# Own terms and keys computed a tile ahead, powers of 1/w beside the squares, another home for half of the rows, smaller gate groups

## The reference

```python
# attention: B=2, H=8 heads, S=768, D=48
for t in range(S):
    cur = np.einsum('bhd,bhe->bhde', u[None] * kt, vt)
    y[:, :, t] = np.einsum('bhd,bhde->bhe', rt, state + cur)
    state = w[None, :, :, None] * state + np.einsum('bhd,bhe->bhde', kt, vt)
# experts: N=1536 tokens of 384, E=8, F=1024
expert_idx = np.argmax(x @ w_gate, axis=1)      # slot = number of earlier tokens of the same expert
h = np.maximum(np.einsum('ecd,edf->ecf', disp, w1), 0.0)
y = np.einsum('ecf,efd->ecd', h, w2)            # out[i] = gate * y[expert, slot]
# last: h = x @ w_in; solu = h * softmax(h); layer norm; @ w_out
```

## Time and profile before

| | us |
|---|---|
| median of 3 runs (lowest, highest) | 366.83 (365.44, 366.9) |
| profiled execution, whole | 366.17 |
| its span (first to last instruction) | 364.4 |
| busy: PE, DVE, ACT, POOL | 330.9, 200.9, 194.0, 189.9 |
| first product of expert 0 | 115.14 |

### The profile page before, as it was taken

The page is one execution under the profiler, slowest core; times in us unless marked ns, Lnnn a source line. Parts: engine busy times, 40 slices in busy tenths (PEclk is TensorE's granted clock), DMA queues, the critical chain, the costliest instruction groups (busy, mean ns, idle before and its releaser), DMA issues.

```text
span 364.4 us, 6469 instructions
## 1 busy us (share of the span) xinstructions
PE 330.9 (91%) x2390; PEld 290.8 (80%) x2390; DVE 200.9 (55%) x444; ACT 194.0 (53%) x372; POOL 189.9 (52%) x170
## 2 busy tenths in 40 slices
PE   5599997886758999999999999999899999999992
PEld 2388886775415999999999999977799999999992
DVE  4346644643362455564546556479966666665640
ACT  2365744756302768666676866645644444444430
POOL 6674757762176758869797885960111111111131
PEclk9879998998858999999999999999999999999998
DMA  8968879991029619485674949400000000000001
GB/s 147 270 191 216 249 178 274 285 345 44 20 82 233 192 27 322 155 289 178 207 247 148 338 142 318 188 4 0 3 22 23 22 22 23 22 23 22 23 25 40
DMA packets 62833, 50.64 MB, mean 139 GB/s; under 512 B 42448, under 2 KB 58192, under 8 KB 62800
## 3 DMA queue, kind: packets, MB, share of 16 engines
q1 hardware_dynamic: 58864, 45.25, 41.1%
q0 software_dynamic: 1920, 4.73, 3.5%
q10 hardware_dynamic: 2016, 0.21, 0.5%
HBM read 38.37 MB, written 11.82 MB: 138 GB/s over the span
## 4 chain that ended last, share of the span: by engine, by line
PE 72%; DVE 7%; issue 6%; POOL 5%; DMA 4%; ACT 4%; SPq 0%; POOLq 0%; DVEq 0%; ACTq 0%
PE ps L1143 23%; PE ps L1393 14%; PE ps L1379 11%; PE ps L1144 11%; PE ps L1402 3%; ACT scores L648 2%; PE ps L1270 2%; PE ps L1285 2%; DMA v_in<-in_v_dram 2%; DMA x_slots<-place,slot 2%; PE ps L1242 1%; PE ps L1265 1%; DMA rows_in<-x_slots 1%; PE ps L1137 1%; POOL place L507 1%
## 5 line engine op out<-in xcount | busy, mean ns | idle before, releaser
L438 POOL TENSOR_TENSOR w_lo<-w_raw,w_hi 128x768 fp32r<-128x768 f32 x32 | 58.6, 1858 | 23.0 <-DVE w_lo L444 22.9
L1143 PE MATMUL ps<-xe,w_hi 128*128 128x448 f32 x192 | 61.7, 377 | 0.3
L1143 PE MATMUL ps<-h,w_hi 128*128 128x448 f32 x192 | 61.6, 377 | 0.0
L1393 PE MATMUL ps<-w_hi,h 128*128 128x384 f32 x192 | 51.8, 340 | 0.3 <-issue 0.3
L1144 PE MATMUL ps<-h,w_lo 128*128 128x224 f32 x192 | 50.8, 264 | 0.0
L1144 PE MATMUL ps<-xe,w_lo 128*128 128x224 f32 x192 | 50.8, 264 | 0.0
L1379 PE MATMUL ps<-w_hi,xe 128*128 128x512 f32 x144 | 46.5, 392 | 0.5 <-DVE xe L1046 0.5
L816 DVE TENSOR_TENSOR ps<-ps,rk_in 128x448 f32<-128x448 f32 x32 | 20.2, 632 | 37.8 <-ACT rk_in L606 37.8
L1143 PEld LDWEIGHTS ps<-xe,w_hi 128*128 128x128 f32 x192 | 36.0, 187 | 5.3 <-issue 2.6
L444 POOL TENSOR_TENSOR w_lo<-w_raw,w_hi 128x1024 fp32r<-128x1024 f32 x16 | 38.2, 2406 | 1.9 <-DVE w_lo L444 1.9
L1143 PEld LDWEIGHTS ps<-h,w_hi 128*128 128x128 f32 x192 | 36.0, 188 | 2.6
(11 more groups left out here) (143 smaller groups left out, 661.0 us busy)
## 6 DMA issues: line engine op xcount, KB each, us to landing
w_raw<-in_moe_w_dram SPq DMA_DIRECT2D x16, 1536.0 KB, 7.6
x_slots<-zeros SPq DMA_DIRECT2D x6, 768.0 KB, 5.0
rk_in<-in_r_dram SPq DMA_DIRECT2D x12, 192.0 KB, 3.0
rk_in<-in_k_dram SPq DMA_DIRECT2D x12, 192.0 KB, 3.6
v_in<-in_v_dram SPq DMA_DIRECT2D x12, 192.0 KB, 4.2
out_dram<-zeros SPq DMA_DIRECT2D x1, 2304.0 KB, 13.5
rows_in<-x_slots SPq DMA_DIRECT2D x8, 192.0 KB, 7.6
w_raw<-in_moe_w_in_dram SPq DMA_DIRECT2D x1, 1536.0 KB, 6.1
```

The costliest lines, as they stand in the source:

```text
L438: eng.tensor_tensor(w1_lo[:, :, cols], w1_raw[:, i, :, cols], w1_hi[:, :, cols].bitcast(F32), ALU.subtract).then_inc(g.w1_lo, 1)
L1143: pe.matmul(ps[:, bank, 0:2 * n], w_hi, x[:, c, 0:2 * n], start=first, stop=False, skip_group_check=True)
L1393: last = pe.matmul(ps[:, OB + i, 0:DM], ht[:, f, i * P:(i + 1) * P], wt[:, f, :], start=(f == 0 and z == 0), stop=(f == KF - 1 and z == 2))
```

## The change

1. r and k of a tile have a semaphore without v; v has its own.
2. POOL does keys (`last_keys`) and own terms (`own_parts`) of tile t+1 in step t, with the state's decay between them, and the scatters behind them. DVE sums the own terms of tile t+2 at the end of step t. ACT writes the diagonal of t+1 before it copies the keys of t+1, and takes x last. The diagonal has a count for each half of the heads.
3. `wsq` also holds powers of 1/w, each the reciprocal of a square; `wpow` starts at 1/w and doubles downwards, in one loop with the squares.
4. Rows of x of batch 1 lie in the second w2 buffer, so taking x waits for no scatter. That buffer's first load moves behind the rows of experts 0 and 1.
5. Groups are tiles 0-2, 3-5, 6-8, 9, 10, 11; two scatters at most per step, from four steps after a group's last tile. Group 4 is counted before the last split of x. One part of w1 is rounded in each of the last four steps instead of two in two.
6. DVE does the routing sums before its remainders of w1, and these wait until all scatters are issued (`scatters_issued`).

```diff
+        def x_rows(t):
+            return x_first[:, t, :] if t < NC else w2_raw[:, 1, t - NC, :]
...
-        GROUPS = [range(0, 4), range(4, 8), range(8, 11), range(11, 12)]
+        GROUPS = [range(0, 3), range(3, 6), range(6, 9), range(9, 10), range(10, 11), range(11, 12)]
         HB, OB, TB = 0, 4, 6
...
                     sp.dma_start(rk_in[:, i, j, :, 0:D], src[b, c]).then_inc(loaded[i], 16)
-                sp.dma_start(v_in[:, i, :, 0:D], v_v[b, c]).then_inc(loaded[i], 16)
+                sp.dma_start(v_in[:, i, :, 0:D], v_v[b, c]).then_inc(v_loaded[i], 16)
...
-            load_w2(1, 1)
...
-            for c in range(NC):
-                sp.wait_ge(scattered[c], 16 * B)
+            sp.wait_ge(scattered, 16 * NT)
             load_rows(0, 0)
             for e in range(E - 1):
                 i = e % 2
                 reach(sp, usual.xe_turned, e)
                 load_rows(e + 1, 1 - i)
+                if e == 0:
+                    load_w2(1, 1)
...
+            def own_parts(t):
+                i = t % NB
+                pool.wait_ge(loaded[i], 32 * (t // NB + 1))
+                if t > 0:
+                    pool.wait_ge(own_step, 2 * t)
+                pool.tensor_tensor(ru[:], rk_in[:, i, 0, :, 0:D], u_all[:], ALU.mult).then_inc(own_step, 1)
+                pool.wait_ge(own_step, 2 * t + 1)
+                if t > 0:
+                    pool.wait_ge(own_ready, t)
+                pool.tensor_tensor(ruk[:], ru[:], rk_in[:, i, 1, :, 0:D], ALU.mult).then_inc(own_step, 1)
+            def last_keys(t):
+                i = t % NB
+                pool.wait_ge(loaded[i], 32 * (t // NB + 1))
+                if t >= 2:
+                    pool.wait_ge(k_turned, t - 1)
+                    pool.wait_ge(update_done, updates(t - 2))
+                pool.tensor_tensor(k_last[:, t % 2, :, 0:D], rk_in[:, i, 1, :, 0:D], wlast[:], ALU.mult)\
+                    .then_inc(k_last_ready, 1)
+            pool.wait_ge(u_in, 16)
+            own_parts(0)
+            pool.wait_ge(wlast_ready, 1)
+            last_keys(0)
+            last_keys(1)
+            own_parts(1)
             pool.iota(token[:, :, 0], pattern=[[P, NT]], base=0, channel_multiplier=1).then_inc(token_ready, 1)
             pool.memset(no_token[:, :, 0], 1 << 20).then_inc(no_token_ready, 1)
             pool.memset(no_token[:].bitcast(F32)[:, :, 1], 1.0).then_inc(no_token_ready, 1)
...
```

The rest of the POOL loop, then ACT and DVE:

```diff
-            for t in range(NT):
+            for t in range(1, NT):
...
-                pool.wait_ge(loaded[i], 48 * (t // NB + 1))
...
-                pool.tensor_tensor(k_last[:, t % 2, :, 0:D], kt, wlast[:], ALU.mult).then_inc(k_last_ready, 1)
...
-                pool.tensor_tensor(ru[:], rt, u_all[:], ALU.mult).then_inc(own_step, 1)
...
-                pool.tensor_tensor(ruk[:], ru[:], kt, ALU.mult).then_inc(own_step, 1)
+                if t < NT - 1:
+                    last_keys(t + 1)
                 if c > 0:
-                    pool.wait_ge(state_ready, m)
+                    pool.wait_ge(state_ready, (NC - 1) * b + c)
                     if t >= 2:
                         pool.wait_ge(y_done, t - 1)
-                    pool.tensor_tensor(state_dec[:, c % 2], state[:], wsq[:, :, 7:8].to_broadcast([P, HP, DP]), ALU.mult)\
+                    pool.tensor_tensor(state_dec[:, c % 2], state[:], wsq[:, 0, :, 7:8].to_broadcast([P, HP, DP]), ALU.mult)\
                         .then_inc(state_dec_ready, 1)
+                if t < NT - 1:
+                    own_parts(t + 1)
                 for _ in range(2):
-                    if any(stored in g and t >= g[-1] + 3 for g in GROUPS):
-                        pool.wait_ge(slots_zeroed, 16 * ZERO_PARTS)
+                    if t >= GROUPS[group_of(stored)][-1] + 4:
+                        if stored == 0:
+                            pool.wait_ge(slots_zeroed, 16 * ZERO_PARTS)
                         scatter(stored)
                         stored += 1
             for t in range(stored, NT):
                 scatter(t)
+            pool.sem_inc(scatters_issued, 1)
...
                     act.wait_ge(y_done, t - 1)
-                for h in range(H):
-                    last = act.activation(scores[:, t % 2, h % 2, h // 2, :], ident[:], ACT.Copy, scale=own[:, h:h + 1])
-                last.then_inc(diag_ready, 1)
+                for a in range(2):
+                    for p in range(HP):
+                        last = act.activation(scores[:, t % 2, a, p, :], ident[:], ACT.Copy,
+                                              scale=own[:, 2 * p + a:2 * p + a + 1])
+                    last.then_inc(diag_ready, 1)
...
-                b, c = divmod(t, NC)
                 act.wait_ge(logits_ready, t + 1)
-                if b > 0:
-                    act.wait_ge(scattered[c], 16 * b)
-                act.activation(x_rows[:, c, :].rearrange("p (q n) -> p q n", q=HP), pairs_of_x()[:, :, 0:2 * D], ACT.Copy)\
+                act.activation(x_rows(t).rearrange("p (q n) -> p q n", q=HP), pairs_of_x()[:, :, 0:2 * D], ACT.Copy)\
...
             for t in range(NT):
                 if t > 0:
                     take_y(t - 1)
+                if t < NT - 1:
+                    put_diagonal(t + 1)
+                    take_k(t + 1)
+                if t > 0:
                     take_x(t - 1)
-                if t < NT - 1:
-                    take_k(t + 1)
-                    put_diagonal(t + 1)
                 for n, g in enumerate(GROUPS):
                     if t == g[-1] + 2:
                         gate_exp(n)
-                if NT - 3 <= t < NT - 1:
-                    act_w1_hi(act, 0, usual.w1_in[0], 16, usual.w1_hi, parts=[2 * (t - NT + 3), 2 * (t - NT + 3) + 1])
-                elif t == NT - 1:
-                    act_w2_hi(act, 0, usual.w2_in[0], 16, usual.w2_hi, parts=[0])
+                if t >= NT - W1_PARTS:
+                    act_w1_hi(act, 0, usual.w1_in[0], 16, usual.w1_hi, parts=[t - NT + W1_PARTS])
             take_y(NT - 1)
+            gate_exp(len(GROUPS) - 2)
+            act_w2_hi(act, 0, usual.w2_in[0], 16, usual.w2_hi, parts=[0])
             take_x(NT - 1)
-            for n in range(len(GROUPS) - 2, len(GROUPS)):
-                gate_exp(n)
+            gate_exp(len(GROUPS) - 1)
             act_w2_hi(act, 0, usual.w2_in[0], 16, usual.w2_hi, parts=[1])
...
-            dve.reciprocal(wpow[:, :, 0:1], wsq[:, :, 7:8]).then_inc(table_step, 1)
+            dve.reciprocal(wsq[:, 1, :, 0], wsq[:, 0, :, 0]).then_inc(inverse_step, 1)
+            dve.wait_ge(inverse_step, 1)
+            dve.tensor_copy(wpow[:, :, P - 1:P], wsq[:, 1, :, 0:1]).then_inc(table_step, 1)
             for j in range(7):
                 n = 1 << j
-                dve.wait_ge(table_step, 8 + j)
-                dve.tensor_tensor(wpow[:, :, n:2 * n], wpow[:, :, 0:n], wsq[:, :, j:j + 1].to_broadcast([P, HP, n]),
-                                  ALU.mult).then_inc(table_step, 1)
+                if j > 0:
+                    dve.wait_ge(square_step, j)
+                dve.tensor_tensor(wsq[:, 0, :, j + 1], wsq[:, 0, :, j], wsq[:, 0, :, j], ALU.mult).then_inc(square_step, 1)
+                dve.wait_ge(table_step, j + 1)
+                dve.wait_ge(inverse_step, j + 1)
+                dve.tensor_tensor(wpow[:, :, P - 2 * n:P - n], wpow[:, :, P - n:P],
+                                  wsq[:, 1, :, j:j + 1].to_broadcast([P, HP, n]), ALU.mult).then_inc(table_step, 1)
+                if j < 6:
+                    dve.wait_ge(square_step, j + 1)
+                    dve.reciprocal(wsq[:, 1, :, j + 1], wsq[:, 0, :, j + 1]).then_inc(inverse_step, 1)
             dve.wait_ge(k_turned, 1)
             dve.wait_ge(wrev_step, 8)
             dve.tensor_tensor(k_dec[:], ps[:, KT, :].rearrange("p (h t) -> p h t", t=P), wrev[:], ALU.mult)\
                 .then_inc(k_first_ready, 1)
-            dve.wait_ge(table_step, 15)
+            dve.wait_ge(table_step, 8)
             decay_r(0)
             dve.wait_ge(desc_ready, 2)
...
+                    dve.wait_ge(diag_ready, 2 * t)
                 dve.tensor_reduce(own[:], ruk[:], AX_X, ALU.add).then_inc(own_ready, 1)
             def mask_scores(t):
-                dve.wait_ge(diag_ready, t + 1)
                 for a in range(2):
+                    dve.wait_ge(diag_ready, 2 * t + a + 1)
                     dve.wait_ge(scores_done, 2 * t + a + 1)
...
-                if t < NT - 1:
-                    add_own(t + 1)
+                if t == 0:
+                    add_own(1)
                 if c < NC - 1:
                     new_state(b, c)
...
+                if t < NT - 2:
+                    add_own(t + 2)
+            place_tokens(len(GROUPS) - 2)
+            add_picked(len(GROUPS) - 2)
             take_logits(NT - 1)
-            for n in range(len(GROUPS) - 2, len(GROUPS)):
-                if n == len(GROUPS) - 1:
-                    pick_experts(n)
-                place_tokens(n)
-                add_picked(n)
```

(14 more changed lines are left out.)

61 lines of the change are left out of this document (23 added, 38 removed).

## The result

The changed kernel takes 348.76 us (median of 4 runs, 347.95 to 350.64), the kernel before, on the same chip, 366.87 (4 runs, 365.44 to 367.03). The ratio is 0.9522, 95% interval 0.9477 to 0.9567. The profiled execution took 348.98, its span is 347.3. The forecast was 347.5, range 344.5 to 355.5. In the experiments further down, two of the four runs of experiment 11 (354.7 and 357.06) and one of the six of experiment 12 (349.47) are slow ones, over 1.5% above the fastest of their kernel, and the medians there contain them.

The account below looks back on a forecast made before the run. TensorE was taken as the bound of the steps, with expert 0's start the question; the last scatter landing at 88.3 instead of 107.65 gave 366.17 - 19.35 = 346.8 profiled, median 347.5 us, range 344.5 to 355.5.

Parts of the forecast that it names:

- Step 1 starts at 17.5: Start: six POOL products, DVE sum, ACT diagonal and key copy let step 1 start at 17.5 us, before 19.6.
- Step 2 starts at 25.4: Start: step 2 begins at 25.4 us instead of 26.8, bounds 24.5 to 26.8.
- rival C: Start wins nothing, key copy behind diagonal and clock low for longer: step 2 at 26.8, total 348.9; chance 0.10.
- The forecast of 7.9: Step 1's start to step 2's: about 7.9 us instead of 5.69, with about 4.4 us at half clock.
- TensorE is the bound: Steps 2 to 10: TensorE sets the time, 5.69 us per full step, step 5 5.08, step 6 4.67.
- Rival B: POOL or DVE bounds the second batch; steps 6 to 10 take 6.7 us each, total 352.5; chance 0.22.
- rival E: Slower: ring of state, decay, own products, sum and mask with POOL and DVE blocking, 369 at 7.9 a step; chance 0.03.
- The load of tile 11: Keys land at 68.9 us, step 11 starts 0.9 late, ACT adds 1.0; bounds of the item 0 to 4.
- a descriptor of 1.0: Tail: last scatter's descriptor takes 0.97 instead of 3.97 us, as DVE's subtractions now wait until scatters are issued.
- rival D: Tail: last descriptor stays at 4 us for a reason of its own, 3.0 more, total 350.5; chance 0.07.
- Everything behind stays: After the last scatter lands: reading the rows, 4.87 us, and everything behind it unchanged.
- the zeros put there: From expert 0 on: second expert's w2 load and POOL's held token writes cost 0; rest of span unchanged, 249 us.

Follow-up runs that it names:

- experiment 11: Changed kernel with old groups, second batch's x rows, DVE's w1 remainders and load_w2(1, 1) in their old places; 354.52 us, ratio 0.9665 to the kernel before.
- experiment 12: Kernel of experiment 9 with 2 instead of 8 TensorE warm-ups between overflow flag and wait for the scatters; 344.99 us, ratio 0.9398 to the kernel before.
- experiment 2: Changed kernel with the old gate groups of 4, 4, 3 and 1 tiles; 350.35 us, ratio 0.9561 to the kernel before.
- experiment 4: Changed kernel with DVE's w1 remainders directly behind the last slot, ahead of the routing sums, no wait for scatters; 351.51 us, ratio 0.9591 to the kernel before.
- experiment 5: Changed kernel with loads of tiles 10 and 11 each issued ahead of the big weight load before them; 346.19 us, ratio 0.9458 to the kernel before.
- experiment 8: Changed kernel with POOL's scatters of a step ahead of its keys, state decay and own products; 349.02 us, ratio 0.9531 to the kernel before.
- experiment 10: Changed kernel with 32 unused bytes behind the table wsq in SBUF; 348.0 us, ratio 0.9494 to the kernel before.
- experiment 1: Kernel before, with only DVE's w1 remainders moved behind the routing sums and a wait for the last scatter's issue; 363.3 us, ratio 0.9925.
- experiment 6: Changed kernel, start reordered: POOL's own products of tile 1 before its keys, ACT's key copy before diagonal 1; 347.91 us, ratio 0.9501 to the kernel before.
- experiment 9: Changed kernel with the edits of experiment 5 and experiment 6 together; 343.05 us, ratio 0.9325 to the kernel before.
- experiment 7: Kernel before, with only the second expert's w2 load moved behind the reading of the rows; 367.16 us, ratio 1.0015.

## Why the prediction was right, and where it was off

*Step starts.* "Step 1 starts at 17.5": it was 18.37. The chain was right, its first link late: w at 5.2, 0.7 of it, and a first own product 0.3 longer. Neither stood in a row of before.

*"Step 2 starts at 25.4".* 26.60 in the profiled execution; rival C, no gain, would be read from it. But six experiments have the same code up to there (2, 4, 5, 8, 10, 11), and five of them have step 2 at 25.4 to 25.7, one at 26.5. From step 1 to step 2 these seven take 7.05 to 8.23 us, because the clock comes back at different moments. The forecast of 7.9 was inside; one profile could not have told C from A. Where 25.4 did come, it came by two errors that cancel: step 1 at 18.2 to 18.5, late by 0.7 to 1.0, and 7.05 to 7.28 from there.

*"TensorE is the bound", steps 2 to 9.* Right to 0.3 us. Step 5 took 5.08 and step 6 4.68, as forecast. Rival B, a second batch bound by POOL or DVE, is refuted by the 44.05 of 44.05; rival E, the ring, too.

*The load of tile 11.* The mis-sized term. I took 68.9 for the landing, "nearer to the row" of 70.7, and bounds of 0 to 4 for the whole item with 1.9 as its value. The landing did not move forward at all (71.2), step 11 started 2.0 late, the late keys then cost 0.6 more, where I had 1.0 for ACT, and the half clock, which was not in the item, 1.0 (experiments 4, 5, 8 and 10): 3.6. The bound held, the choice in it was too hopeful: the request came 2.3 earlier, but behind 1.5 MB of weights the load did not. What rival B named, "DVE's own sum now standing ahead of the mask", was seen here too: it cost TensorE 1.37 us, in step 10 alone and for want of the load.

*The tail.* "a descriptor of 1.0" was right, and so was its reason for the kernel before (experiment 1); rival D and the Trainium skill's inference with it are refuted for that place. But the price is not a constant: 3.97 with DVE's group begun 0.76 us before the descriptor, 1.44 with it begun 0.36 before (experiment 4), 0.98 with it begun 0.05 behind (experiment 11). The end of step 11 to the end of the descriptor took 5.6 where I had 5.0.

*"Everything behind stays."* Reading the rows took 6.0 us from the landing of the scatter to the first product instead of 7.5. This gain of 1.5 was not forecast; without it the total would have been 2.8 us off instead of 1.3. It belongs to this execution more than to the change. From the first issue of the rows to the first product it took 7.4 us before and 6.0 here, and 6.3 to 7.7 in experiments 2, 5, 6, 8, 9, 10 and 11, which run the same 16 warm-ups; here alone they ran at full clock, in 3.62 us. Why the rows themselves landed sooner is not shown, only that the load of w2 is not it (experiment 7). From expert 0 on the span is 249.8 against 249.3, and 249.3 to 249.8 in all twelve experiments: the zeros put there were right.

So the total was right to 0.4% by a sum of errors of both signs: +1.2 at the start, +1.0 in the steps up to 11, +0.5 in step 11, +0.6 in the tail, -1.5 at the rows, +0.5 behind. Between the two profiled executions it was 2.2 us off (348.98 against 346.8); the rest closed because the forecast added 0.7 to come to the median, and the median of the change lies 0.2 below its profiled execution.

## What to carry to other kernels

Once every engine works a step ahead, look for what cannot be moved ahead by order alone: here a small load queued behind a big one, which swallowed a gain of 3 us and a loss of 2 us, with next to nothing left of either in the time. Parts of a change that remove the same wait (small groups, a DVE group moved away) are each worth it alone (4.8 and 3.2 us here) and little on top of each other: with everything else in place the groups were worth 0.7 to 1.4, and the descriptor of experiment 11 took 0.98 with the DVE group not moved. So price them in both contexts. And where a time comes out as a theory says, read the row that the theory speaks of before believing it.
